# Beginning TensorE's buffers on 2048-byte boundaries in a fused convolution and two-MLP kernel

## The reference

```python
w = softmax(weight, axis=-1)                       # (8 heads, 7 taps)
x_pad = concatenate([zeros(B, 6, D), x], axis=1)
x_unf = x_pad[:, idx, :].reshape(B, S, 7, 8, 24)   # idx[s, k] = s + k
y = einsum('hk,bskhg->bshg', w, x_unf).reshape(B * S, D)
h = y @ moe_w_in;   g = maximum(0.01 * h, h);      y = g @ moe_w_out
h = y @ moe2_w_in;  g = where(h >= 1, h, where(h <= -1, 0, (h + 1) ** 2 / 4))
out = g @ moe2_w_out
```

## Time and profile before

| | before |
|---|---|
| median of 3 runs | 1140.1 us |
| the profiled execution | 1139.77 us |
| its span | 1138.0 us |
| PE busy | 1126.9 us, 99% |
| PEld busy | 922.7 us |
| DVE busy | 897.3 us, 79% |
| ACT busy | 797.8 us, 70% |
| mean granted TensorE clock | 0.999 |

### The profile page before, as it was taken

The page is one execution under the profiler, slowest core; times in us unless marked ns, Lnnn a source line. Parts: engine busy times, 40 slices in busy tenths (PEclk is TensorE's granted clock), DMA queues, the critical chain, the costliest instruction groups (busy, mean ns, idle before and its releaser), DMA issues.

```text
span 1138.0 us, 25723 instructions
## 1 busy us (share of the span) xinstructions
PE 1126.9 (99%) x9754; PEld 922.7 (81%) x9754; DVE 897.3 (79%) x1511; ACT 797.8 (70%) x1472; POOL 50.3 (4%) x76
## 2 busy tenths in 40 slices
PE   7999999999999999999999999999999999999998
PEld 6788888888888888888888888888888888888886
DVE  7787877888777887788877788787787877888665
ACT  6768767586775867758577685866758667686685
POOL 5533000000000000000000000000000000000000
PEclk9999999999999999999999999999999999999999
DMA  6330000101001010010100101001010100100001
GB/s 142 97 80 2 14 16 1 29 2 25 5 1 30 1 29 1 1 29 1 29 1 8 23 1 29 1 13 18 1 29 1 24 7 1 29 1 15 1 1 28
DMA packets 114569, 21.98 MB, mean 19 GB/s; under 512 B 106257, under 2 KB 114449, under 8 KB 114449
## 3 DMA queue, kind: packets, MB, share of 16 engines
q1 hardware_dynamic: 111600, 19.61, 9.4%
q10 hardware_dynamic: 2848, 0.75, 0.3%
HBM read 14.05 MB, written 6.29 MB: 18 GB/s over the span
## 4 chain that ended last, share of the span: by engine, by line
PE 93%; DVE 3%; ACT 2%; issue 1%; DMA 0%; DVEq 0%; ACTq 0%
PE hidden L417 14%; PE acc_edge L475 10%; PE acc_main L481 10%; PE acc_main L483 10%; PE acc_main L485 10%; PE hidden L413 10%; PE hidden L415 10%; PE hidden L411 10%; PE acc_edge L472 10%; DVE g_lo L951 1%; DVE g L940 0%; ACT g_hi L682 0%; DVE acc_main L887 0%; ACT pre L670 0%; DVE acc_main L851 0%
## 5 line engine op out<-in xcount | busy, mean ns | idle before, releaser
L682 ACT CAST g_hi<-g 128x512 fp32r<-128x512 f32 x510 | 299.2, 618 | 280.2 <-PE acc_main L513 214.4
L951 DVE TENSOR_TENSOR g_lo<-g,g_hi 128x512 fp32r<-128x512 f32 x510 | 335.0, 690 | 104.1 <-ACT g_hi L682 99.3
L945 DVE SCALAR_TENSOR_TENSOR g<-hidden,pre 128x512 f32<-128x512 f32 x256 | 176.7, 690 | 105.9 <-ACT pre L670 100.5
L417 PE MATMUL hidden<-op_edge,w_edge 64*128 64x512 f32 x768 | 257.3, 388 | 0.0
L411 PE MATMUL hidden<-op_hi,w_main 64*128 64x512 f32 x512 | 198.9, 389 | 3.2 <-DVE g L940 1.7
L429 PE MATMUL hidden<-op_hi,w_main 64*128 64x512 f32 x512 | 199.2, 389 | 0.0
L433 PE MATMUL hidden<-op_hi,w_main 64*128 64x512 f32 x512 | 198.9, 388 | 0.0
L413 PE MATMUL hidden<-op_lo,w_main 64*128 64x512 f32 x512 | 198.8, 388 | 0.0
L438 PE MATMUL hidden<-op_edge,w_edge 64*128 64x512 f32 x512 | 198.7, 388 | 0.0
L431 PE MATMUL hidden<-op_lo,w_main 64*128 64x512 f32 x512 | 198.7, 388 | 0.0
L415 PE MATMUL hidden<-op_hi,w_main 64*128 64x512 f32 x512 | 198.7, 388 | 0.0
(11 more groups left out here) (128 smaller groups left out, 2778.2 us busy)
## 6 DMA issues: line engine op xcount, KB each, us to landing
x_in<-in_x_dram SPq DMA_DIRECT2D x67, 64.0 KB, 2.3
out_dram<-y_main SPq DMA_DIRECT2D x62, 64.0 KB, 1.8
stage<-in_moe_w_out_dram SPq DMA_DIRECT2D x15, 192.0 KB, 2.7
x_in_edge<-in_x_dram SPq DMA_DIRECT2D x66, 32.0 KB, 1.9
out_dram<-y_edge SPq DMA_DIRECT2D x32, 64.0 KB, 1.8
stage<-in_moe_w_in_dram SPq DMA_DIRECT2D x15, 128.0 KB, 2.3
stage<-in_moe_w_in_dram SPq DMA_DIRECT2D x30, 64.0 KB, 2.3
stage<-in_moe_w_out_dram ACTq DMA_DIRECT2D x1, 192.0 KB, 4.0
```

The source lines that it names most:

```text
L417: done = nc.tensor.matmul(h[:], w_edge[l][top, i - 3, cols], op_edge[l][b][top, :], start=False, stop=False)
L682: nc.scalar.copy(hi_of(n, c)[:], g[c % SLOTS][:]).then_inc(g_hi_ready, 1)
L951: nc.vector.tensor_tensor(lo_of(n, c)[:], g[c % SLOTS][:], hi_of(n, c)[:].bitcast(F32), ALU.subtract).then_inc(g_lo_ready, 1)
```

## The change

The SBUF buffers are named in another order. First come `taps` and `x_edge[0]`, then a filler `to_line` that ends at a multiple of 2048 bytes, then everything that fp32r matmuls read: `w_main`, `w_edge`, `w_out`, the four kinds of `op_` buffers, `g_hi` and `g_lo`. Each of these has a size that is a multiple of 2048 bytes, so each begins on such a multiple. The other buffers follow. `taps_raw` to `own_taps`, used only while the taps are made, are no longer buffers of their own but parts of `y_main`. No instruction is added, removed or moved.

```diff
+LINE = 2048
+FIRST_FREE = 16512
...
+        taps = sb("taps", [P, 2, TAPS])
+        x_edge = [sb("x_edge0", [P, HALO + HALF])]
+        sb("to_line", [P, (LINE - FIRST_FREE % LINE - 64 - 1056) // 4])
         w_main = [sb(f"w_main{l}", [P, 2, F], F32R) for l in (0, 1)]
         w_edge = [sb(f"w_edge{l}", [P, 2, F], F32R) for l in (0, 1)]
         w_out = [sb(f"w_out{l}", [P, CHUNKS, 2 * D], F32R) for l in (0, 1)]
-
-        stage = [sb(f"stage{i}", [P, 2 * PW + PC * D]) for i in range(AHEAD)]
-
-        taps_raw = sb("taps_raw", [P, H, TAPS])
...
-        own_taps = sb("own_taps", [P, 2, H, TAPS])
-        taps = sb("taps", [P, 2, TAPS])
...
-        x_edge = [sb(f"x_edge{b}", [P, HALO + HALF]) for b in (0, 1)]
-
         op_hi = [[sb(f"op_hi{l}{b}", [P, T], F32R) for b in (0, 1)] for l in (0, 1)]
         op_lo = [[sb(f"op_lo{l}{b}", [P, T], F32R) for b in (0, 1)] for l in (0, 1)]
         op_edge = [[sb(f"op_edge{l}{b}", [P, T], F32R) for b in (0, 1)] for l in (0, 1)]
         op_top = [[sb(f"op_top{l}{b}", [P, T], F32R) for b in (0, 1)] for l in (0, 1)]
+        g_hi = [sb(f"g_hi{i}", [P, T], F32R) for i in range(SLOTS)]
+        g_lo = [sb(f"g_lo{i}", [P, T], F32R) for i in range(SLOTS)]
+        x_edge.append(sb("x_edge1", [P, HALO + HALF]))
+        stage = [sb(f"stage{i}", [P, 2 * PW + PC * D]) for i in range(AHEAD)]
...
+        used = 0
+
+        def in_y_main(*shape):
+
+            nonlocal used
+            first, used = used, used + math.prod(shape)
+            part = y_main[:, first:used]
+            if len(shape) == 1:
+                return part
+            if len(shape) == 2:
+                return part.rearrange("p (a b) -> p a b", b=shape[1])
+            return part.rearrange("p (a b c) -> p a b c", b=shape[1], c=shape[2])
+
+        taps_raw = in_y_main(H, TAPS)
...
+        own_taps = in_y_main(2, H, TAPS)
```

More of the change, by code:

```diff
@@ L13 @@
+import math
 from contextlib import ExitStack
@@ L87, in bass_conv_mlp_mlp @@
         w_out = [sb(f"w_out{l}", [P, CHUNKS, 2 * D], F32R) for l in (0, 1)]
-        stage = [sb(f"stage{i}", [P, 2 * PW + PC * D]) for i in range(AHEAD)]
-        taps_raw = sb("taps_raw", [P, H, TAPS])
[L92 to L99, removed]
-        own_taps = sb("own_taps", [P, 2, H, TAPS])
-        taps = sb("taps", [P, 2, TAPS])
-        x_in = [sb(f"x_in{b}", [P, T]) for b in (0, 1)]
-        x_in_edge = [sb(f"x_in_edge{b}", [P, HALF]) for b in (0, 1)]
-        x_main = [sb(f"x_main{b}", [P, HALO + T]) for b in (0, 1)]
-        x_edge = [sb(f"x_edge{b}", [P, HALO + HALF]) for b in (0, 1)]
         op_hi = [[sb(f"op_hi{l}{b}", [P, T], F32R) for b in (0, 1)] for l in (0, 1)]
@@ L114, in bass_conv_mlp_mlp @@
         op_top = [[sb(f"op_top{l}{b}", [P, T], F32R) for b in (0, 1)] for l in (0, 1)]
+        g_hi = [sb(f"g_hi{i}", [P, T], F32R) for i in range(SLOTS)]
+        g_lo = [sb(f"g_lo{i}", [P, T], F32R) for i in range(SLOTS)]
+        x_edge.append(sb("x_edge1", [P, HALO + HALF]))
+        stage = [sb(f"stage{i}", [P, 2 * PW + PC * D]) for i in range(AHEAD)]
+        x_in = [sb(f"x_in{b}", [P, T]) for b in (0, 1)]
+        x_in_edge = [sb(f"x_in_edge{b}", [P, HALF]) for b in (0, 1)]
+        x_main = [sb(f"x_main{b}", [P, HALO + T]) for b in (0, 1)]
         conv_main = sb("conv_main", [P, T])
@@ L119, in bass_conv_mlp_mlp @@
         g = [sb(f"g{i}", [P, T]) for i in range(SLOTS)]
-        g_hi = [sb(f"g_hi{i}", [P, T], F32R) for i in range(SLOTS)]
-        g_lo = [sb(f"g_lo{i}", [P, T], F32R) for i in range(SLOTS)]
         edge_b = sb("edge_b", [EDGE, T])
@@ L126, in bass_conv_mlp_mlp @@
         y_edge = sb("y_edge", [EDGE, T])
+        used = 0
[9 more added lines that the diff above has]
+        taps_raw = in_y_main(H, TAPS)
+        taps_max = in_y_main(H)
+        taps_sub = in_y_main(H, TAPS)
+        taps_exp = in_y_main(H, TAPS)
+        taps_sum = in_y_main(H)
+        taps_den = in_y_main(H)
+        taps_inv = in_y_main(H)
+        own = in_y_main(3, H)
+        own_inv = in_y_main(2, H)
+        own_taps = in_y_main(2, H, TAPS)
         hidden = [psum(f"hidden{i}") for i in range(SLOTS)]
```

## The result

The changed kernel took 1130.07 us (median of 6 runs, 1129.76 to 1131.47); the kernel before, in the same measurement, 1140.36 us (median of 6 runs). One of these six, at 5722 us, was disturbed; without it the median is 1140.24 us. The ratio is 0.9912, with a 95% interval of 0.9899 to 0.9926: faster by 0.9%, or 10 us, where 60 were forecast.

A forecast was written before the change was run, and what follows sets the result against it. PE's matmul rate was taken to bound the kernel, with 12.5 ns a slot blamed on addresses: 1139.77 - 60.8 for the buffers' order + 1 for stalls gave 1080 us; range 1072 to 1142.

The forecast's parts named there:

- What bounds the kernel: Whole run: PE busy 99% of the span, so TensorE's matmul rate, 228.9 ns a slot, sets the end, not waits.
- fast case: All fp32r slots: the address costs all 12.5 ns, so time falls to 1080 us, range 1074 to 1090; chance 0.50.
- The order of the buffers: Stream addresses in every fp32r slot: gain between nothing and 12.5 ns a slot; 60.8 us taken as likeliest.
- three reasons for the far end: For 60.8 us: excess equal at offsets 192 and 1216, exact from slot to slot, near one more 128-byte piece (13.3 ns).
- The format, not the address: Fp32r streams: the 12.5 ns come from twice the bytes, wherever they begin; no change, 1140 us; chance 0.37.
- likeliest case: Whole run: 1139.77 less 60.8 plus 1 us for stalls, 1080 us; chance 0.50.
- Colliding starts: Weight loads and streams both starting on multiples of 512 meet in memory, lengthening slots; 1201 us at 12.5 ns more; chance 0.08.
- PE freed, but the others bind: End of smooth jobs: address helps, but ACT and DVE don't follow; 1 us stall a pair, 1095 us; chance 0.05.
- The weights' loads: Weight loads before each matmul: crossing costs at most 3 ns, hidden under the matmul before; cost and gain zero.
- Vector, scalar and DMA addresses: Moved buffers of the other engines: at most 5 ns between like DVE operations, costing nothing thanks to idle time.
- The temporaries: Taps' temporaries in `y_main`: done at 6.35 us, first written over at 135.62, so no wait added; zero.
- What is late next: End of smooth jobs, `g` and `g_lo`: some 0.37 and 0.39 us of slack remain; 1 us added for the run.

The follow-up runs named there:

- the first kernel of matmuls: Matmuls alone, no other engine working, changing one thing per group: stream place, weights' place, column count or format; excess over streaming 13.3 ns at 256, 384 and 512 columns.
- the kernel with 215.8 ns: Kernel before, streams read with halves in turn, all reordering in the first layer's operand, every sixteenth column first; 1099.73 us, ratio 0.9644.
- the swapped order: Streams read as columns 0, 256, 2, 258, ... then 1, 257, ...; on the kernel before 1140.24 us, on the changed kernel 1129.88 us.

## Why the prediction was wrong

**What bounds the kernel** was right. PE's rate sets the end, and nearly the whole change is in it: 2.2 ns in each of 4864 slots. That 1130 us lies within the stated 1072 to 1142 is no merit of the prediction: the range joins a fast case (1074 to 1090) and a case of no change (1137.8 to 1142.4), and 1130 is in neither. Two jobs were to take 65.8 or 69.6 us, and they take 68.91. It wrote down the two bounds of the address's share, 0 and 12.5 ns, but gave no chance to a value between them.

**The order of the buffers** is the step that failed, in its size and in its cause. It gave the address 12.5 ns a slot, 60.8 us; the address has 2.2 ns, 10.8 us by the slots and 10 us by the clock. Of the three reasons for the far end, the first was misread: the excess is equal for streams at 192 and 1216 because both are 64 away from the weights modulo 256, not because both run over a boundary. The second (the same in every slot) holds, and is as true of a price that every stream in order pays. The third, the guess of 128-byte pieces, fell with the first kernel of matmuls: at distances 128 and 192 the step is longer, at 256 as short as at 0. The prediction compared with `x_edge`'s matmuls and saw two differences, bytes and address, to one of which all 12.5 ns had to belong. They are divided: 2.2 go with the address. The other 11 go with fp32r streams read in order; the same 2048 bytes read from two halves in turn cost none of it, and the order of reading is a cause that the prediction never listed.

A page of the Trainium skill, "TensorE: Matmul & The Clock Gate", section "Step-by-step: what each phase is for", says that loading the next weights doesn't take read bandwidth from the running matmul. The runs differ from it for fp32r: the load's place alone moves a step from 226.7 to 232.4 or 233.4 ns. For bf16 three places of the stream (0, 64 and 1536) gave the same 215.9.

**The rivals.** *The format, not the address* was nearer to the measured time, 10 us off where the likeliest case was 50 off. Its account of 11 ns holds for streams read in order, but it forecast no change. *Colliding starts* had the right kind of mechanism with the sign turned: load and stream do disturb each other, and starts at the same place modulo 256 are, at 512 columns, the best case found. At distances 128 and 192 it is a loss of 18 and 20 us, so the unforecast danger of this change was real. *PE freed, but the others bind* did not arise in the change itself: the waits of PE in the jobs stayed at 2.3 us.

**The weights' loads** cost nothing, as said: 182 to 185 ns before and after, and a weight slice over a multiple of 2048 steps at 226.7. **Vector, scalar and DMA addresses**: DVE and ACT are busy within 0.6 us of before. **The temporaries**: nothing, shown by the run of them alone.

**What is late next** could be tested only in the kernel with 215.8 ns. The place was right (the end of smooth jobs, `g_lo` and `g` late). The size was not: 1 us was forecast for the whole run, 8 as the far end of the fast case and 16 in the rival. That kernel gives (34.29 - 32.83) = 1.5 us in this pair of jobs; over the run, its 1098.5 us of span are some 24 us more than 1138.0 - 4864 x 13.1 ns = 1074.3. It also makes DVE's operations at chunks 7 and 8 slower (`op_lo` 1056 ns and 682 before). In this pair three of them take 2.3 us, 1.5 before, just ahead of a `g` for which ACT's chain waits (2.21 us of idle at 646.11). So how much of the 1.5 us a kernel without that would show stays open.

**What stays open** is the mechanism: why distance 0 is best, why 28 equals it and 4 and 4 does not, why a step can settle in two ways, why halves in turn avoid the excess when the swapped order doesn't.

## What to carry to other kernels

When every instruction of an engine has the same small excess, change one address at a time in a kernel of matmuls alone before moving buffers: it costs one run and would have given the right size here. Where fp32r weights and streams of 512 columns are read in order, place them so that their starts are equal modulo 256 bytes, all of them; half of it, or a chance distance, cost up to 1.9% against distance 64 and 2.7% against distance 0. For other lengths measure first: at 256 columns distance 64 was better. An even excess that isn't contention may still be the order's: fp32r streams read from two halves in turn ran 5 to 6% faster, and pay if the reordering is put where few operations do it.

## What the runs showed of the hardware

- A step of 512 fp32r columns takes from 226.7 to 240.0 ns (distance 20) by the places of stream and weights alone, at equal loads and granted clock. bf16 of 512 and plain f32 of 256 columns take 215.8 to 215.9. With 256 fp32r columns distance 0 takes 119.8 to 120.0 and distance 64 takes 117.8.
- The same 512 columns take 215.8 ns with halves in turn (at distances 0 and 64), 333 with pairs in turn, 487 with eight parts in turn.
- Reordering from SBUF slows ACT and DVE. A cast of 618 ns became 885 with its input read 8 bytes apart and 1145 with its output written 1024 bytes apart; DVE's subtraction went from 690 to 827 and 1131, in the second case with its `g_hi` input read 1024 bytes apart as well. Inputs 16 bytes apart cost 1343 ns for ACT's copy of `edge_sum` (619 before) and 1510 for DVE's `op_lo` (682 before); 64 bytes apart, `op_lo` took 1056. From PSUM, reading 16 bytes apart was free: ACT's cast of `acc_main` to `op_hi` stayed at 586 ns, DVE's subtraction from `acc_main` at 671.
